# Block 0 passes group C5 alone before the pair's turn; T parts over more chunks, B4's backs in five banks, a low part after a mix

## What is computed

```python
def reference(**kwargs):
    attn_out = _attn_ref(**attn_kwargs)            # 2 x 8 heads, 768 positions, head size 64, window 128 + 4 sinks
    x = attn_out.transpose(0, 2, 1, 3).reshape(B * S, H * D)       # 1536 tokens x 512
    x = _moe_ref(x, w_gate, w_val, w_out)          # "B": 512 -> 1536 -> 512
    return _moe2_ref(x, w_in, w_out, alpha)        # "C": 512 -> 2048 -> 512

def _moe_ref(x, w_gate, w_val, w_out):
    g = x @ w_gate
    return (g * (1.0 / (1.0 + np.exp(-g))) * (x @ w_val) @ w_out)

def _moe2_ref(x, w_in, w_out, alpha):
    h = x @ w_in
    return ((np.maximum(h, 0.0) + alpha * np.minimum(h, 0.0)) @ w_out)
```

## Time and profile before

| | us |
|---|---|
| median of 3 runs | 647.74 (647.62 to 647.92) |
| the profiled execution | 647.59 |
| its span, first to last instruction | 645.9 |

### The profile page before, as it was taken

The page is one execution under the profiler, slowest core; times in us unless marked ns, Lnnn a source line. Parts: engine busy times, 40 slices in busy tenths (PEclk is TensorE's granted clock), DMA queues, the critical chain, the costliest instruction groups (busy, mean ns, idle before and its releaser), DMA issues.

```text
span 645.9 us, 9455 instructions
## 1 busy us (share of the span) xinstructions
PE 625.1 (97%) x3072; PEld 489.1 (76%) x3072; DVE 410.7 (64%) x696; ACT 244.9 (38%) x585; POOL 445.3 (69%) x592
## 2 busy tenths in 40 slices
PE   8889999999999999999999999997999999999998
PEld 5567676776776888878787878875788888888886
DVE  5945667556575866464647474987766765647474
ACT  4635553644544632121312020445523443315160
POOL 7848688896976889898989385599997785500000
PEclk9999999999999999999999999998999999999999
DMA  9343333312221002120212221001111201000004
GB/s 301 103 148 115 116 107 106 132 35 65 97 84 50 17 34 81 50 65 34 66 37 67 92 66 50 17 2 65 66 65 66 83 17 66 1 0 1 1 10 186
DMA packets 28815, 44.62 MB, mean 69 GB/s; under 512 B 2816, under 2 KB 8960, under 8 KB 28768
## 3 DMA queue, kind: packets, MB, share of 16 engines
q1 hardware_dynamic: 28624, 43.76, 20.8%
q10 hardware_dynamic: 144, 0.26, 0.1%
HBM read 40.87 MB, written 3.15 MB: 68 GB/s over the span
## 4 chain that ended last, share of the span: by engine, by line
PE 79%; POOL 7%; DVE 6%; issue 4%; ACT 4%; DVEq 0%; POOLq 0%; ACTq 0%
PE ffn_ps L1962 25%; PE att_ps L1936 20%; PE ffn_ps L1877 12%; PE att_ps L1962 7%; PE ffn_ps L1936 5%; PE att_ps L1826 2%; PE att_ps L1788 2%; POOL w_lo L1649 2%; PE att_ps L1805 1%; DVE scratch L2189 1%; POOL w_lo L1677 1%; ACT scratch L2004 1%; POOL scratch L1703 1%; PE att_ps L1969 1%; POOL w_hi L1648 1%
## 5 line engine op out<-in xcount | busy, mean ns | idle before, releaser
L1649 POOL TENSOR_TENSOR w_lo<-raw_weights,w_hi 128x512 fp32r<-128x512 f32 (+1 forms) x124 | 149.8, 1208 | 9.9
L1648 POOL CAST w_hi<-raw_weights 128x512 fp32r<-128x512 f32 (+1 forms) x124 | 77.0, 621 | 37.6 <-PE ffn_ps L1962 12.9
L2305 DVE TENSOR_TENSOR scratch<-ffn_ps,scratch 128x512 f32<-128x512 f32 x112 | 76.5, 687 | 36.7 <-PE ffn_ps L1962 36.1
L1677 POOL TENSOR_TENSOR w_lo<-part_sum,w_hi 128x256 fp32r<-128x256 f32 x80 | 63.8, 797 | 6.4
L1877 PE MATMUL ffn_ps<-x_hi,w_hi 128*128 128x512 f32 x152 | 61.7, 406 | 2.0 <-DVE x_lo L2326 1.0
L1877 PE MATMUL ffn_ps<-x_hi,w_lo 128*128 128x512 f32 x152 | 59.4, 391 | 0.0
L1877 PE MATMUL ffn_ps<-x_lo,w_hi 128*128 128x512 f32 x152 | 59.2, 390 | 0.0
L1729 POOL TENSOR_TENSOR scratch<-scratch,inv 128x264 f32<-128x264 f32 (+1 forms) x48 | 31.4, 655 | 31.9 <-DVE inv L2178 31.6
L1962 PE MATMUL ffn_ps<-h_hi,w_hi 128*128 128x512 f32 x128 | 50.8, 397 | 0.0
L1962 PE MATMUL ffn_ps<-h_hi,w_lo 128*128 128x512 f32 x128 | 49.9, 390 | 0.0
L1962 PE MATMUL ffn_ps<-h_lo,w_hi 128*128 128x512 f32 x128 | 49.8, 389 | 0.0
(11 more groups left out here) (207 smaller groups left out, 1578.3 us busy)
## 6 DMA issues: line engine op xcount, KB each, us to landing
raw_weights<-pieces SPq DMA_DIRECT2D x118, 256.0 KB, 2.7
k_sb<-kt SPq DMA_DIRECT2D x12, 264.0 KB, 3.4
v_sb<-vt SPq DMA_DIRECT2D x12, 256.0 KB, 2.7
out<-scratch SPq DMA_DIRECT2D x12, 256.0 KB, 2.0
q_sb<-qt SPq DMA_DIRECT2D x11, 256.0 KB, 3.4
scratch<-vs SPq DMA_DIRECT2D x1, 384.0 KB, 5.1
q_sb<-qt ACTq DMA_DIRECT2D x1, 256.0 KB, 2.7
alpha<-alpha_t SPq DMA_DIRECT2D x1, 8.0 KB, 6.3
```

The costliest lines, as they stand in the source:

```text
L1648: chain(pool.tensor_copy(hi, raw[:, r % n_raw, at]))
L1649: last = pool.tensor_tensor(lo, raw[:, r % n_raw, at], hi.bitcast(F32), ALU.subtract)
L1677: pool.tensor_tensor(lo, s, hi.bitcast(F32), ALU.subtract).then_inc(split_done, 1)
L2305: ins = dve.tensor_tensor(total, back_ps(key), total, ALU.add)
```

## The change

Five edits. (1) `n_alone` is 6 in place of 5: C5 passes block 0 alone as well. (2) After the last back of C3 and the fronts of C4 come the fronts of C5 and the backs of C4 before the first strip of C0; the backs of C5 take the place of C4's between the strips of C0 and C1. Behind them C6 is the first shared group. (3) T's high and low parts no longer come as a pair after one chunk each; `high_after` and `low_after` name the chunk after which each stands, from chunk 2 to chunk 16 of the new list `turn`, the low part one or two chunks behind its high part. (4) The last eight backs of B go through banks (2, 3, 4, 0, 1, 2, 3, 4) in place of (2, 0, 1, 2, 0, 1, 2, 0). (5) In B's second part the low part of hidden tile (1, 1) comes one chunk later.

```diff
-    n_alone = 5
+    n_alone = 6
...
-                emit(chunk, now, *([[("hidden", h12), ("rest", h21)], [("rest", h12)]] if i == 6 else []))
+                emit(chunk, now, *([[("hidden", h12)], [("rest", h21)], [("rest", h12)]] if i == 6 else []))
...
-    steps = [[("thi", key), ("tlo", key)] for key in parts_of_sums("C")]
...
-    for n, chunk in enumerate(backs(groups_c[3]) + fronts(groups_c[4])):
+    turn = (backs(groups_c[3]) + fronts(groups_c[4]) + fronts(groups_c[5]) + backs(groups_c[4]) + strips(groups_c[0], 0))
+    steps = parts_of_sums("C")
+    low_after = dict(zip((4, 5, 6, 8, 10, 14, 15, 16), steps))
+    high_after = dict(zip((2, 4, 5, 6, 8, 12, 13, 15), steps))
+    for n, chunk in enumerate(turn):
         emit_chunk(chunk)
-        if n >= 2 and steps:
-            plan += steps.pop(0)
-    waiting = backs(groups_c[4])
+        if n in low_after:
+            plan.append(("tlo", low_after[n]))
+        if n in high_after:
+            plan.append(("thi", high_after[n]))
+    waiting = backs(groups_c[5])
     for g in groups_c:
-        for chunk in strips(g, 0):
-            emit_chunk(chunk)
-            if steps:
-                plan += steps.pop(0)
+        if g != groups_c[0]:
+            for chunk in strips(g, 0):
+                emit_chunk(chunk)
...
-                home = (rest_of_b if g != pair_b[-1] else (2, 0, 1, 2, 0, 1, 2, 0))[4 * (t - 1) + d]
+                home = (rest_of_b if g != pair_b[-1] else (2, 3, 4, 0, 1, 2, 3, 4))[4 * (t - 1) + d]
```

## The result

| | before | after |
|---|---|---|
| median of the runs, us | 647.68 (646.07 to 647.92, 4 runs) | 639.59 (639.26 to 640.56, 4 runs) |
| ratio, with its 95% interval | | 0.9883 (0.9864 to 0.9902) |
| the profiled execution | 647.59 | 640.56 |
| its span | 645.9 | 638.8 |
| from the first start after attention to the last matmul's start | 437.54 | 430.16 |

The changed kernel is 8.1 us faster by the medians, 7.0 by the two profiled executions. The last three lines of the table are worked out from PE's starts as in the prediction: a hole is the distance of two starts less 0.227, restart and slow steps included.

A forecast was written before the change was run, and what follows sets the result against it. PE was taken as busy throughout except for holes: 8.3 us in the turn, 1.84 in B. Gains of 6.4 in the turn and 1.6 in B, 8.0 us, gave a median of 639.7 us, range 637.7 to 642.8.

The forecast's parts named there:

- low clock: Turn, ten steps from 442.80 us at the 1.2 GHz level: the 1.61 us lost there go without 5 us of standstill.
- Edits 1 to 3: Turn, C5 ahead of C0's strips: keep's hole of 1.58 us goes, mix 0's 3.47 becomes 0.2, the clock's 1.61 goes.
- The banks: Turn, C3's backs: the first back's hole goes, 0.8 + 0.08 us comes at the fourth; gain 0.2 to 0.3.
- the bound of 1.1: Upper bound, in us, on the gain from the new banks at C3's backs; the lower was 0.
- Edit 5: B, before strip 3 in four gaps: a low part goes behind mix 0, gain 1.6 us, bounds 0 and 1.84.
- mix 0 then comes 0.60 earlier: B, DVE: moving one low part behind mix 0 brings mix 0 forward by that part's 0.60 us start to start.
- The bound of 0: B: no gain from moving the low part if the time before mix 0 stretches otherwise.
- The prediction's own test: The forecast is wrong if B's holes stay, or if the T sums start later than B4's evac allows.
- What was added: Turn: C5's second front stalls 0.3 us; POOL splits 7.2 us more, C1's sums at 444.5; T sums start as before.
- The pile-up: Turn, DVE's low parts at 1.79 us beside POOL: up to 4 us reach PE, about 643 us; chance 0.20.
- that rival: Turn, 425 to 448: short stalls bring the 1.2 GHz level and it stays, up to 657.7 us; slower, chance 0.03.
- Closing all holes but C1's: Turn and B: all holes close, C3's fourth back too, 9.7 us gained, 638.0 us; chance 0.08.

The follow-up runs named there:

- e3_parts_paired: The changed kernel with edit 3 alone undone, T's high and low parts in pairs again, one pair a chunk; 644.49 us, ratio 0.9943.
- e4_order_only: The kernel before with T's parts spread over the strips of C0, C5 left shared, old banks and old B; 649.38 us, ratio 1.0009.
- e5_low_only: The kernel before with edit 5 alone; 646.75 us, ratio 0.9984 (0.9963 to 1.0004).
- e1_low_undone: The changed kernel with edit 5 alone undone, the low part of tile (1, 1) again ahead of mix 0; 640.70 us, ratio 0.9877.

## Why the prediction was right, point by point

The forecast was 639.7 us (637.7 to 642.8), the median 639.59. The terms, in us left after the change:

| place | before | forecast | measured |
|---|---|---|---|
| C3's backs | 1.11 | 0.88 | 0 |
| second front of C5 | – | 0.3 | 0.34 |
| strip 2, the keep | 1.66 | 0 | 0 |
| strip 3, mix 0 | 3.47 | 0.2 | 0 |
| low clock | 1.61 | 0 | 0 |
| strip 1 of C1 | 0.46 | 0.46 | 0.63 |
| B's four gaps | 1.84 | 0.24 | 1.63 |
| sum | 10.15 | 2.1 | 2.6 |

- **Edits 1 to 3** were right in mechanism and size: keep, mix 0 and clock gave 6.7 us where 6.5 were forecast, and `e3_parts_paired` and `e4_order_only` show that both halves are needed for all of it. The clock's 1.61 is the size of the profiled execution and not of each: 3 of the 37 executions of the kernel before that ran beside the experiments had a granted clock of 1.000 and took 646.5 to 646.8 us, the other 34 had 0.994 to 0.997 and took 647.4 to 650.8. In after mix 0 ends at 446.8 against the forecast 448.0; the low parts of T took 1.04 us on the average in place of 1.27.
- **The banks** were the step that failed to the good side. The forecast kept 0.8 us at C3's fourth back, because it took the earlier trace rows's 3.39 us for two low parts of x as something that the change doesn't move. They took 2.51, the evac behind them ended at 424.9, and PE asked at 425.1. PE asked only 0.2 us behind that end, so this is in part luck. The same stretching that the prediction counted on elsewhere was taken here as fixed; the bound of 1.1 was the right end. Measured worth: 1.2.
- **Edit 5** failed to the bad side: 1.6 us forecast, 0.1 measured, and 1.26 on the kernel before. The failed step is "mix 0 then comes 0.60 earlier". It comes 0.38 earlier, since it must wait for the product. By 0.38 a gap the kernel before would gain 1.4, near the 1.26 of `e5_low_only`. The rest is POOL's phase, the instants at which its instructions start against DVE's. Taken from the instant at which PE asks for strip 3, the product starts 0.94 us ahead in after and 1.85 ahead in `e1_low_undone` at the second gap, 1.39 and 1.84 at the first, and 1.27 and 1.28 at the last, where edit 5 does save 0.34. The bound of 0 named "if the time before mix 0 stretches otherwise", and so it was. The prediction's own test, that it is wrong if B's holes stay, was met for this term.
- **What was added** was as free as forecast: POOL 6.5 us busier against 7.2, its sums for C1 done at 448.8 for strips from 460 on (4.3 us later than the forecast 444.5, and at no cost), the T sums started by B4's evac after 3.69 us idle, the second front of C5 at 0.34. There the cause given, relu and T's part on ACT, is a near second: it ends 0.3 us ahead of the low part on DVE, and the run with that part moved shows that the low part holds the bank.
- **The rivals.** The pile-up did not come in the changed kernel; it is what `e3_parts_paired` ran into. The clock did not fall in the profiled executions of after, where no hole is longer than 0.8 us. The argument against that rival, that the clock fell only after 5 us idle, was too easy: it also fell behind 1.18 and 2.61 us (`e3_parts_paired`) and behind 2.78 (`e4_order_only`). Closing all holes but C1's, 638.0, is near what moving two or three parts more then gave: 638.7 to 638.9 with two low parts, 638.0 with the high part as well.
- **The total** agreed better than its terms. The turn gave 7.3 for 6.4, B 0.2 for 1.6. The sum of the holes is 0.5 above the forecast. In the profiled execution attention ended 0.3 later than in that of before and the matmuls took 0.2 more, so it read 640.56, 1.0 above the forecast 639.6 for it. The median of after lies 1.0 below its profiled execution. That this brought the median to within 0.1 is chance.

What stays open: why POOL meets DVE at other instants in B when only instructions elsewhere, or one behind a mix, have moved. The phase was the same in both profiled executions of the changed kernel, and nothing here traced it back to its start.

## What to carry to other kernels

When work jams at a turn, two things have to come together for the whole gain: other work for the engine that waits, and an order in which the jammed instructions don't stand ahead of those that this other work hangs on. Either alone left or made holes of 1.2 to 2.9 us at another place here. Where the waiting instruction would directly follow one that it depends on, count the end of that one and not its start-to-start distance. And where an engine's instructions are held up by another engine's, a margin of a few tenths of a microsecond is no margin; here moving a whole instruction out of the way closed the holes.

## What the runs showed of the hardware

- A 128x512 DVE instruction with both inputs in SBUF took 0.68 to 1.78 us, by when a POOL instruction that reads SBUF, a CAST included, started. A stretched one ended 0.55 us behind POOL's, all 8 times in B's pair. For the low part of a hidden tile of B the mean was 1.08 us beside POOL's subtractions and 0.72 without them. It can be POOL's that is stretched instead, 1.29 to 1.62, and a start 0.04 us earlier turned one case into the other.
- Two DVE instructions of 128x512 with an operand in PSUM followed each other at 0.60 us, and at 0.82 when the second has to wait for the end of the first.
- In the profiled executions TensorE kept its 2.4 GHz level through single holes of up to 1.03 us. It fell to the 1.2 GHz level (starts 0.43 apart) behind two of 1.58 and 3.39 (before), behind two of 1.18 and 2.61, and behind one of 2.78; there a second hole of 2.93 us followed, and the starts were 0.43 apart for 5.7 us more. So the spread without C5 cost 3.4 us more than its holes in that execution. Executions of one kernel differ in it: of `e3_parts_paired` one of six had a granted clock of 0.997, the others 0.999 or 1.000.
- Three rows name POOL as the releaser where the other rows point to DVE: strip 1 of C1 in the earlier trace rows, 439.72 in `e3_parts_paired`, and 441.44 in `e4_order_only`, where POOL had ended at 440.78 and DVE's low part at 441.34. For strip 1 of C1 the changed kernel shows it, where the hole went when the low part alone was moved; the other two are read from the rows.
